# Pooled attention outputs of the later batches: added to x by GpSimd, features on partitions, in place of DMAs and VectorE

## What is computed

```python
q_d = q.reshape(B, H, Sd, 4, D).mean(axis=3)          # k_d, v_d alike; Sd = 144
out_up = np.repeat(sm_attn(q_d, k_d, v_d), 4, axis=2)  # softmax over 144 pooled keys
scores = np.where(abs(i - j) < 4, scale * q @ k.T, -1e9)
x = out_up + softmax(scores) @ v                       # -> (2304, 512)
g = np.maximum(x @ w_in, 0) ** 2                       # 512 -> 2048
x2 = g @ w_out                                         # 2048 -> 512
h = max(x2 @ w1, x2 @ w2, x2 @ w3)                     # 512 -> 768
out = h @ w_out2                                       # 768 -> 512
```

## Time and profile before

| | |
|---|---|
| median of 3 runs | 823.77 us (823.2 to 826.59) |
| the profiled execution, its own time | 823.62 us |
| its span in the profile | 821.9 us |
| TensorE busy | 798.3 us, 97%, 5715 instructions |
| VectorE busy | 450.4 us, 55% |
| ScalarE busy | 329.3 us, 40% |
| GpSimd busy | 242.6 us, 30% |
| the low part of G on GpSimd | 128 instructions, mean 1.06 us |
| chain that ended last | TensorE 86%, VectorE 6%, DMA 3%, ScalarE 2% |
| mean granted clock of TensorE | 0.996 of full |

### The profile page before, as it was taken

One profiled execution on the slowest core, in us unless ns is written; L12 is line 12 of the kernel. 1 busy time (PEld: TensorE's weight loads), 2 busy tenths in 40 slices (PEclk: granted clock), 3 DMA queues, 4 the chain that ended last, 5 costly groups with the idle time before them and its releaser, 6 DMA issues.

```text
span 821.9 us, 13821 instructions
## 1 busy us (share of the span) xinstructions
PE 798.3 (97%) x5715; PEld 770.8 (94%) x5715; DVE 450.4 (55%) x510; ACT 329.3 (40%) x888; POOL 242.6 (30%) x215
## 2 busy tenths in 40 slices
PE   8999999999899999799999999999999999999996
PEld 7898999999899999699999999999999999999996
DVE  5668878899678999469790059221312222121211
ACT  5786664545654545553545433211112112121111
POOL 6677632448623466412453233000000000000000
PEclk9999999999999999999999999999999999999999
DMA  8992310132300323200000155210201101010101
GB/s 175 269 273 56 89 45 1 25 88 60 94 1 6 84 51 87 69 2 12 33 30 2 48 174 154 68 39 10 68 1 39 39 17 60 1 39 1 25 16 38
DMA packets 52751, 49.06 MB, mean 60 GB/s; under 512 B 23400, under 2 KB 44680, under 8 KB 51920
## 3 DMA queue, kind: packets, MB, share of 16 engines
q1 hardware_dynamic: 50116, 47.45, 21.4%
q10 hardware_dynamic: 2572, 0.73, 0.4%
HBM read 36.81 MB, written 10.32 MB: 57 GB/s over the span
## 4 chain that ended last, share of the span: by engine, by line
PE 86%; DVE 6%; DMA 3%; ACT 2%; SPq 1%; issue 1%; ACTq 0%; POOL 0%; DVEq 0%
PE PS L669 26%; PE PS L671 25%; PE PS L670 25%; PE PS L916 1%; PE PS L711 1%; DVE sc L1299 1%; SPq L523 1%; DMA vb<-v 1%; PE PS L694 1%; DMA qk<-q 1%; DVE qk L1352 1%; DVE tmp L1290 1%; DMA WOr<-k 1%; PE PS L718 1%; PE PS L702 1%
## 5 line engine op out<-in xcount | busy, mean ns | idle before, releaser
L669 PE MATMUL PS<-XS,WI 128*128 128x288 f32 (+1 forms) x768 | 242.6, 316 | 0.0
L670 PE MATMUL PS<-XS,WI 128*128 128x288 f32 (+1 forms) x768 | 238.0, 310 | 0.0
L671 PE MATMUL PS<-XS,WI 128*128 128x288 f32 (+1 forms) x768 | 238.0, 310 | 0.0
L1800 POOL TENSOR_TENSOR G<-g,G 128x288 fp32r<-128x288 f32 x128 | 136.0, 1064 | 231.2 <-ACT G L1097 230.8
L669 PE MATMUL PS<-G,WO 128*128 128x288 f32 x512 | 154.9, 303 | 3.9 <-POOL G L1800 3.7
L670 PE MATMUL PS<-G,WO 128*128 128x288 f32 x512 | 151.4, 296 | 0.0
L671 PE MATMUL PS<-G,WO 128*128 128x288 f32 x512 | 151.2, 295 | 0.0
L669 PEld LDWEIGHTS PS<-XS,WI 128*128 128x128 f32 x768 | 144.4, 188 | 4.1 <-issue 2.5
L670 PEld LDWEIGHTS PS<-XS,WI 128*128 128x128 f32 x768 | 145.1, 189 | 1.3
L671 PEld LDWEIGHTS PS<-XS,WI 128*128 128x128 f32 x768 | 144.8, 189 | 0.0
L1092 ACT ACTIVATE PS<-PS 128x288 f32<-128x288 f32 x128 | 50.9, 398 | 147.3 <-PE PS L671 133.9
(11 more groups left out here) (189 smaller groups left out, 1159.8 us busy)
## 6 DMA issues: line engine op xcount, KB each, us to landing
x_scratch<-x2s SPq DMA_DIRECT2D x8, 576.0 KB, 3.5
XR<-x_scratch SPq DMA_DIRECT2D x6, 768.0 KB, 4.9
out<-osb SPq DMA_DIRECT2D x15, 256.0 KB
qk<-q SPq DMA_DIRECT2D x6, 576.0 KB, 5.3
qk<-k SPq DMA_DIRECT2D x3, 1152.0 KB, 7.7
vb<-v SPq DMA_DIRECT2D x3, 1152.0 KB, 8.4
WOr<-moe_w_out SPq DMA_DIRECT2D x6, 512.0 KB, 8.1
WIr<-moe_w SPq DMA_DIRECT2D x12, 256.0 KB, 3.3
```

The lines of the kernel that those rows point to most:

```text
L669: mm(dst, wt(HI), xt_(HI), start=first, stop=False)
L670: mm(dst, wt(HI), xt_(LO), start=False, stop=False)
L671: return mm(dst, wt(LO), xt_(HI), start=False, stop=last)
L1800: Q.tensor_tensor(G[:, s % NGR, LO], g32[:, s % 2], G[:, s % NGR, HI].bitcast(f32), ALU.subtract).then_inc(g_ready, 1)
```

## The change

For the batches 1 to 3 the pooled probabilities are divided by their sum (times 4) before they are transposed. The sums come with the exps as accumulator outputs (`hsum`); VectorE does `heads_normed` for each pair, and t waits for it. The o task has pooled v as the stationary operand and `prT` as the moving one, so that its output has features on partitions, two heads in two column halves; ScalarE copies it to `odT`. There is no `scale_pooled`, no DMA of outputs and no `add_pooled`; `band_out` is raised by the last value step. The x task still transposes the local outputs into `x32`; then GpSimd adds `odT` there (`x_add`, two instructions for each x task), and the high part is split off three places later (`X_LATER`, a plan entry "split"). The places of qk, s, t, o and x tasks change, and the SP queue loads v at the same point in all batches. One task of batch 0, ("P", 5), moves two places later.

```diff
-    QK_PACE, HEADS_PACE, HEAD_AT = 3, 8, (0, 4, 6)
+    QK_PACE, HEADS_PACE, HEAD_AT, X_LATER = 3, 10, (0, 7, 9), 3
-    QK_AT = {1: (0, 14, 1), 2: (2, 14, 3), 3: (4, 12, 3)}
-    HEADS_AT = {1: (1, 1, 0), 2: (3, 1, 0), 3: (4, 14, 3)}
-    X_AT = {1: [(1, 14, 2), (1, 15, 0), (1, 15, 1), (2, 10, 1), (2, 10, 3), (2, 11, 1)],
-            2: [(3, 14, 0), (3, 14, 2), (3, 15, 0), (4, 9, 1), (4, 9, 3), (4, 10, 1)],
-            3: [(5, 12, 3), (5, 13, 3), (5, 14, 3), (6, 9, 1), (6, 10, 1), (6, 11, 1)]}
+    QK_AT = {1: (0, 14, 1), 2: (2, 14, 2), 3: (4, 12, 0)}
+    HEADS_AT = {1: (1, 1, 0), 2: (3, 1, 0), 3: (4, 14, 0)}
+    X_AT = {1: [(1, 12, 2), (1, 13, 1), (1, 14, 0), (2, 9, 3), (2, 10, 2), (2, 11, 1)],
+            2: [(3, 13, 0), (3, 13, 3), (3, 14, 2), (4, 8, 3), (4, 9, 2), (4, 10, 1)],
+            3: [(5, 12, 3), (5, 13, 2), (5, 14, 1), (6, 9, 1), (6, 10, 1), (6, 11, 1)]}
-                 ... ((0, 10, 1), ("P", 5)),
+                 ... ((0, 10, 3), ("P", 5)),
             put(place, 0, b, X[t:t + 1])
+            put(place, X_LATER, b, [("split", t)])
@@ SP queue
-                    if b < NB - 1:
-                        sp.wait_ge(band_out, LAST[b - 1] - 1)
-                        load_v(b)
+                    sp.wait_ge(band_out, LAST[b - 1] - 1)
+                    load_v(b)
                     filled(sp, b - 1, X[-1])
                     load_q(b, 1)
-                    if b == NB - 1:
-                        sp.wait_ge(band_out, LAST[b - 1] - 1)
-                        load_v(b)
-                pooled_out_to_groups(b)
@@ TensorE
                 elif kind == "t":
-                    read(pe, b, ("s", c))
+                    pe.wait_ge(heads_made, KC * (b - 1) + c + 1)
...
-                    for e in range(2):
-                        for n in range(2):
-                            for kn in range(2):
-                                last = mm(heads_o[:, e, n], prT[:, e, kn, q_part(n)], vd[:, kn, 2 * c + e, :], start=kn == 0, stop=kn == 1)
+                    for kn in range(2):
+                        for e in range(2):
+                            last = mm(ps[64 * e:64 * e + 64, :SD], vd[:, kn, 2 * c + e, :D], prT[:, e, kn], start=kn == 0, stop=kn == 1)
@@ ScalarE
-                            last = A(pr[:, e, n, :], heads_s[:, e, n], ACT.Exp, bias=hst[:, 2 * c + e, n:n + 1], scale=-1.0)
+                            last = A(pr[:, e, n, :], heads_s[:, e, n], ACT.Exp, bias=hst[:, 2 * c + e, n:n + 1], scale=-1.0,
+                                     accum_out=hsum[:, 2 * c + e, n:n + 1])
...
-                        act.wait_ge(od_loaded, OD_MOVES * (b - 1))
-                    A(view(od_st[:, 4 * c:4 * c + 4], "p (e n) d -> p e n d", n=2), heads_o, ACT.Copy).then_inc(att_free[bk], 1)
+                        act.wait_ge(x_added, x_count(b - 1, len(X) - 1))
+                    A(odT[:, c], ps[:, :SD], ACT.Copy).then_inc(att_free[bk], 1)
...
-                    read(act, b, task)
+                else:                                  # ("split", t)
+                    done = x_count(b, task[1])
+                    n, at, cnt = x_place(b, task[1])
+                    act.wait_ge(x_added, done)
                     A(xs(n, HI, at, at + cnt), x32[:, done % 2, :, :cnt], ACT.Copy).then_inc(x_hi, 1)
@@ VectorE
+            def heads_normed(b, c):
+                read(dve, b, ("s", c))
+                rec = hsum[:, 2 * c:2 * c + 2]
+                link(V.tensor_scalar(rec, rec, EPS, float(POOL), ALU.add, ALU.mult))
+                link(V.reciprocal(rec, rec))
+                V.tensor_tensor(pr, pr, rec.unsqueeze(3).broadcast_to([SB, 2, 2, SD]), ALU.mult).then_inc(heads_made, 1)
...
+                run(seg, 4)
+                heads_max(b, 0)
+                run(seg, 2)
+                heads_normed(b, 0)
+                run(seg)
+                softmax_in(lo)
+                heads_max(b, 1)
+                softmax_out(lo)
+                seg = value_steps(lo, two)
+                heads_normed(b, 1)
+                run(seg, 3)
+                heads_max(b, 2)
+                run(seg, 2)
+                heads_normed(b, 2)
+                run(seg, 3)
+                heads_max(b, 3)
+                run(seg, 3)
+                heads_normed(b, 3)
+                run(seg)
                 dve.wait_ge(q_loaded[1], 16 * b)
-                scale_pooled(b, 0)
...
-                scale_pooled(b, 1)
-                run(seg, 6)
-                add_pooled(lo)
-                run(seg)
+                run(score_steps(hi, two))
                 softmax_in(hi)
                 softmax_out(hi)
                 run(value_steps(hi, two))
-                add_pooled(hi)
@@ GpSimd
+            def x_add(b, t):
+                read(pool, b, ("x", t))
+                read(pool, b, ("o", KC - 1))
+                x = x32[:, x_count(b, t) % 2].rearrange("p c (i g) -> p c i g", g=NG)
+                units = odT[:].rearrange("p c (g j) -> p c j g", j=NJ)
+                row, end = 2 * XP[t][0], 2 * XP[t][1]
+                at = row
+                while at < end:
+                    stop = min(end, POOL * (at // POOL + 1))
+                    part = x[:, :, at - row:stop - row, :]
+                    unit = units[:, :, at // POOL].unsqueeze(2).broadcast_to([P, KC, stop - at, NG])
+                    last = Q.tensor_tensor(part, part, unit, ALU.add)
+                    at = stop
+                last.then_inc(x_added, 1)
...
                     if task[0] == "x":
+                        x_add(b, task[1])
+                    elif task[0] == "split":
                         x_lo_part(b, task[1])
@@ row_sum of v
-                    pool.wait_ge(od_loaded, OD_MOVES * (b - 1))
+                    pool.wait_ge(vd_stored, 16 * (b - 1))
```

More of the change, by code:

```diff
@@ L145, in attention_and_two_mlps @@
             put(place, 0, b, X[t:t + 1])
+            put(place, X_LATER, b, [("split", t)])
     SEQ = [(0, t) for t in opening if t[0] not in ("block", "add")] + [(0, t) for t in FIRSTS]
[L147 to L152 removed]
+    SEQ += [bt for key in sorted(PLAN) for bt in PLAN[key] if bt[1][0] != "split"]
     ATT = (6, 7, 0, 1, 2, 3, 4, 5)
@@ L673, in attend @@
             def attend(b, task):
+                if task[0] == "split":
+                    return
                 if b == 0:
@@ L1042, in attend @@
                     return second(task)
-                bk = bank_of(b, task)
                 kind = task[0]
-                ps = PS[:, ATT[bk]]
+                if kind != "split":
+                    bk = bank_of(b, task)
+                    ps = PS[:, ATT[bk]]
                 if kind == "qk":
@@ L1350, in value_steps @@
                     dve.wait_ge(dve_step, max(made["product", o], made.get(("acc", o - 1), 0)))
-                    to = acc if o < BAND - 1 else qk[:, lo:hi, :]
-                    made["acc", o] = count(V.tensor_tensor(to, acc, own[o % m], ALU.add))
-                    yield
-                dve.wait_ge(dve_step, steps[0])
-            def add_pooled(n):
-                b, (lo, hi) = BATCH[n], ROWS[n]
-                dve.wait_ge(od_loaded, OD_MOVES * b)
-                j0, j1 = -(-lo // POOL), hi // POOL
-                if lo < POOL * j0:
-                    acc = qk[:, lo:POOL * j0, :]
-                    link(V.tensor_tensor(acc, acc, odg[:, j0 - 1:j0, :].broadcast_to([P, POOL * j0 - lo, D]), ALU.add))
-                if hi > POOL * j1:
-                    acc = qk[:, POOL * j1:hi, :]
-                    link(V.tensor_tensor(acc, acc, odg[:, j1:j1 + 1, :].broadcast_to([P, hi - POOL * j1, D]), ALU.add))
-                acc = view(qk[:, POOL * j0:POOL * j1, :], "p (j t) d -> p j t d", t=POOL)
-                add = odg[:, j0:j1, :].unsqueeze(2).broadcast_to([P, j1 - j0, POOL, D])
-                V.tensor_tensor(acc, acc, add, ALU.add).then_inc(band_out, 1)
-                dve.wait_ge(band_out, n - 1)
+                    ins = V.tensor_tensor(acc, acc, own[o % m], ALU.add)
+                    if o < BAND - 1:
+                        made["acc", o] = count(ins)
+                    else:
+                        ins.then_inc(band_out, 1)
+                        dve.wait_ge(band_out, n - 1)
+                    yield
             def pool_rows(dst, rows):
@@ L1596, in _ @@
                 lo, hi = FIRST[b], LAST[b]
-                if b == 1:
-                    run(seg, 4)
-                    heads_max(b, 0)
-                    run(seg, 4)
-                    heads_max(b, 1)
-                    run(seg)
-                    softmax_in(lo)
-                    softmax_out(lo)
-                    seg = value_steps(lo, two)
-                    run(seg, 3)
-                    heads_max(b, 2)
-                    run(seg, 4)
-                    heads_max(b, 3)
-                    run(seg)
-                else:
+                if b > 1:
                     dve.wait_ge(q_loaded[0], 16 * b)
@@ L1805, in _ @@
                 for place in range(1, PLACES):
```

(2 more changed lines are left out.)

56 lines of the change are left out of this document (11 added, 45 removed), and 2 rows, old and new, of the table SECOND_AT.

## The result

The changed kernel takes 829.96 us (median of 5 runs, 828.73 to 830.96); the kernel before took 825.0 beside it (5 runs, 823.2 to 826.59). The ratio is 1.0061 [1.0046, 1.0075]: 5 us slower, where 9.5 us less were forecast, and outside the range. The profiled execution took 828.73 us, 5.1 more than that of before. It is the fastest of the five and its mean granted clock was 0.995; the other four took 829.78 to 830.96 at 0.988 to 0.990, so the median holds more time at the low clock than the profile shows.

The account below looks back on a forecast made before the run. TensorE, busy 97% of the span and in program order, was taken as the bound. Gains of 19.4 us less new holes of 10.1 gave 9.3, taking 823.62 to 814.3; the 8-in-10 range was 806.5 to 821.

Parts of the forecast that it names:

- I cost it at nothing: GpSimd's x_add, 1.45 us per x task: an overrun of 4.5, about what G may be late by, costed at nothing.
- the third rival: GpSimd's add, split and low part take over if x_add exceeds 1.8 us; at 2.9, 834 us; chance 0.07.
- The second rival: GpSimd's additions slow VectorE, so each heads_normed and the band's softmax come later: 820.1 us; chance 0.12.
- So ... which closes the 1.2 us hole: Batch 0's task (P, 5) moved two places (1.6 us) later, claimed to close a TensorE hole of 1.2 us.
- These hide: Accumulator reads added to four exps on ScalarE, 0.2 us each at most, claimed to cost nothing.
- (1): Fourth t of each batch waits for heads_normed, late by 0.7 to 0.8 us; three batches, 2.4.
- (2): Batch 2, chunk boundary (4,0): third split of x stands behind the band's exp, which waits for VectorE; 2.7 us.
- (3): Batch 3's first qk task waits for pooled q: hole of 3.6 us plus half of 1.7 for the clock, 4.4.
- (4): A hole before the first score of batch 3, 0.6 us.
- The gains: Shorter o tasks (0.30 saved 12 times, 3.6 us) and closed TensorE holes, 19.4 us in all.
- 3.7 + 1.7 at G: Batch 3: earlier load of v closes the 3.7 us hole of late G and the 1.7 of low clock behind it.
- Boundary of batch 1: First-half x transposes of batch 1 come two slots earlier, so the chunk boundary holes of 0.7 + 0.4 us go.

Follow-up runs that it names:

- tiny_add: Changed kernel with x_add cut to one addition over 16 elements per x task, most pooled outputs left out of x: 822.44 us, 0.9972.
- spread2_tiny: spread2 with x_add cut to one addition over 16 elements, most pooled outputs left out of x: 809.36 us, 0.9809.
- x_apart: Changed kernel with first-half x tasks some places earlier and a slot apart, each split four places behind its x task: 823.25 us, 0.9982.
- p5_back: Changed kernel with (P, 5) put back at (0,10,1): 829.97 us, 1.0057.
- heads_later: Changed kernel with the heads of batches 1 and 2 two places later: 829.54 us, 1.0065.
- before_v_early: Kernel before the change, with v also loaded early in the last batch as the only edit: 824.88 us, 0.9999.
- spread: Changed kernel with all three batches on one pattern, splits never preceding squares, two value steps before the fourth normalisation, some exps and row sums later: 821.51 us, 0.9964.
- qk3_later: Changed kernel with batch 3's qk and head tasks three places later, where they stood before the change: 828.62 us, 1.0052.
- exp_later: Changed kernel with the exp of batch 2's second half planned at slot (4,0) instead of (3,15): 828.05 us, 1.0043.
- spread2: spread with first-half x tasks two places earlier and qk of batch 1 at (0,14,1): 815.18 us, 0.9882.

## Why the prediction was wrong

- **"I cost it at nothing" (GpSimd).** This is the step that failed. I had worked out an overrun of 4.5 us against what G may be late by, and let the average decide. The x chain took 5.2 us of holes, and x_add's neighbours slowed down: without it the kernel gains 7.5 us (tiny_add), well placed 5.8 (spread2_tiny). x_add took 1.75 us, and 2.46 where the large hole stands; the third rival, from 1.8 on, was given 0.07 at 834, and its mechanism (split waits for x_add, squares behind) is the one in the timeline at 163.11. It struck at one group heavily and not at all six. That it is the order and not GpSimd's work alone shows in x_apart: with the same additions, and x tasks and splits at other places, the kernel takes 6.7 us less. The shares of a resource say nothing here; the order in two queues does.
- **Contention.** The second rival had it at 0.12. Of its three terms one came, the band's softmax later (1.2 at (4,0), by tiny_add); `heads_normed` did not come later, since t was late by 0.94 with and without the addition. The means don't show it: VectorE's product for the scores (1152 elements) went from 1.47 to 1.68 us but is 1.62 in tiny_add, that for the values fell from 1.68 to 1.51, and G, 1.06 before and 1.15 after, is 1.14 in tiny_add. Single instructions do: x_add is 1.36 us at its shortest, under my 1.45, and 1.75 in the mean. The Trainium skill, SBUF — State Buffer, section "SBUF: two separate sides", says that of a VectorE instruction with two SBUF inputs and a GpSimd instruction that reads SBUF the one that starts first holds the shared ports for its whole length and the other waits. The additions of 16 elements in tiny_add agree: 0.22 us, or until 0.1 us behind the end of VectorE's product. That rule, which spoke against the change, deserved more than a rival's 3 us.
- **"So ... which closes the 1.2 us hole" of (P, 5).** It closed, and TensorE waited 1.5 us at the next thing that VectorE owed it, the low part of w_out behind pool_q: `down` was due 0.4 us sooner than before and that part came 1.1 later. p5_back shows the term is worth 0. VectorE was the limit of both.
- **"These hide" (accumulator reads).** Twice they did not: the exps stand ahead of the copies of x2s in the second slot of a chunk, and with the reads they last 0.4 us longer; t, moved from ahead of that `down` to behind it, gave 0.6 more of the way to a hole of 0.8 each time (heads_later, with the exps behind the copies, has neither hole).
- **Holes (1) to (4).** All four opened where forecast, with the forecast's releaser. (1) was right in size, 0.94 for 0.8. (2), (3) and (4) were too small by 1.1, 1.9 and 0.6. tiny_add closes 1.2 of (2) and 1.2 of (3), but in (3) that isn't why the forecast missed, since it had pool_q at 4.6 and it took 4.8: short were the issue (0.5 behind the transposes), the transfer with its issue (5.6, not 5.05) and the transposes themselves, which ran at the low clock (0.35). The low clock cost 2.6, not 0.8.
- **The gains.** o tasks 0.87 us from start to start against 1.15, so 3.4 of 3.6 (TensorE after, next to its old row):

```profile
115.85 0.71 PE L693 MATMUL PS<-prs,vd 72*64 72x144 f32 x8
```

  The closed holes came as listed. But the gain of 3.7 + 1.7 at G and the loss of 4.4 in hole (3) are two ends of one due time. The forecast kept 1.0 of them as a net gain; before_v_early shows 0.
- **Boundary of batch 1.** 0.7 + 0.4 went, and 2.5 of the x chain came.

Of the 15.6 us between 829.96 and 814.3: x_add with what it slows 7.5; the two missed places and the start 3.9; the rest, some 4, is in the foreseen holes and in the clock. What remains open is why the clock fell for 3.4 us in one run and 6.8 in another at holes of one size: the five runs of the changed kernel are 2.2 us apart, with mean clocks from 0.995 to 0.988.

## What to carry to other kernels

When a kernel has one saturated engine in program order, a closed hole pays only up to the next due time: before counting it, look at what the engine meets next if it comes that much earlier, and count both ends as one term. Work put on a half-idle engine is judged in its queue, by who waits behind whoever waits for it, at the worst instance and not the mean. And try the new placing on the old code: here, with the whole addition in place, it was the whole gain.

## What the hardware showed that I had not expected

- An instruction of GpSimd with little to do that starts beside a product on VectorE lasts until 0.1 us behind that product's end (tiny_add): 128x16 elements 0.22 us beside a reduction or nothing, 0.80 to 1.36 beside a product of two SBUF operands; 128x128 elements 0.51 to 1.68.
- An exp with an accumulator output starts its successor 0.36 us later, though exp and read last 0.37 + 0.19 in the list; the two overlap. Without the read, in the kernel before, it was 0.26.
- The granted clock fell to the 1.2 GHz level behind holes of 2.5 us (spread, three times) and not behind one of 3.0 (x_apart). Nor did it behind the 3.8 at (4,0) in the changed kernel, and it did behind the same 3.8 in qk3_later and p5_back, and behind one of 2.2 in exp_later. So these runs have no length of hole that parts the two, and the forecast's bounds from two rows (3.7: it fell; 2.5: it didn't) don't hold in them. In spread2, with no hole over 1.9 us, it didn't fall; the changed kernel and exp_later had the same hole of 2.5 at 165, and only the second a drop behind it.
